# Splitting the raw weight blocks earlier and starting the block sums behind them, in a transformer kernel on one core

## What is computed

```python
def _moe_ref(x, w_in, w_out):          # w_in 512x2048, w_out 2048x512
    h = x @ w_in
    g = h - np.tanh(h)
    return g @ w_out

def _moe2_ref(x, w_in, w_out, g_ln):   # w_in 512x1024, w_out 1024x512
    h = x @ w_in
    e = np.exp(h - np.max(h, axis=-1, keepdims=True))
    solu = h * (e / (np.sum(e, axis=-1, keepdims=True) + 1e-09))
    mu, var = mean(solu), var(solu)    # over a row
    ln = (solu - mu) / np.sqrt(var + 1e-06) * g_ln
    return ln @ w_out
```

## Time and profile before

| | |
|---|---|
| median of 3 runs | 832.08 us (832.0 to 832.1) |
| the profiled execution | 825.32 us, its span 823.5 us |
| busy share of the span | PE 97%, PEld 84%, DVE 58%, ACT 48%, POOL 34% |
| granted TensorE clock, mean | 0.998 of full speed |

### The profile page before, as it was taken

One profiled execution on the slowest core, in us unless ns is written; L12 is line 12 of the kernel. 1 busy time (PEld: TensorE's weight loads), 2 busy tenths in 40 slices (PEclk: granted clock), 3 DMA queues, 4 the chain that ended last, 5 costly groups with the idle time before them and its releaser, 6 DMA issues. The chain is left out here.

```text
span 823.5 us, 14650 instructions
## 1 busy us (share of the span) xinstructions
PE 800.8 (97%) x4498; PEld 694.6 (84%) x4498; DVE 475.8 (58%) x1101; ACT 394.7 (48%) x935; POOL 280.3 (34%) x322
## 2 busy tenths in 40 slices
PE   6999999998999999999999999998999899999998
PEld 5888888887888888888888888897888788888886
DVE  5889888888854332233223322338678666666662
ACT  5999899888544332222222222325444443433433
POOL 3687787778100000000000000008274744444400
PEclk9999999999999999999999999999999999999999
DMA  7665555545433100000000000000200000000001
GB/s 184 149 154 159 143 137 154 144 114 145 138 113 110 65 1 0 1 1 0 0 0 0 0 0 0 0 1 1 102 1 1 27 25 27 14 25 25 13 25 51
DMA packets 77719, 46.34 MB, mean 56 GB/s; under 512 B 59824, under 2 KB 68144, under 8 KB 77680
## 3 DMA queue, kind: packets, MB, share of 16 engines
q1 hardware_dynamic: 75232, 45.19, 19.3%
q10 hardware_dynamic: 2448, 0.66, 0.4%
HBM read 40.97 MB, written 4.87 MB: 56 GB/s over the span
## 5 line engine op out<-in xcount | busy, mean ns | idle before, releaser
L1450 PE MATMUL psum<-x_hi,w1i 128*128 128x464 f32 (+1 forms) x640 | 185.7, 371 | 0.5 <-DVE w1i L1103 0.5
L1463 PE MATMUL psum<-gate_hi,w1o 128*128 128x464 f32 (+1 forms) x640 | 146.8, 371 | 3.3 <-DVE gate_lo L1146 3.3
L1463 PEld LDWEIGHTS psum<-gate_hi,w1o 128*128 128x128 f32 x640 | 119.9, 188 | 18.0 <-DVE gate_lo L1146 4.4
L1450 PEld LDWEIGHTS psum<-x_hi,w1i 128*128 128x128 f32 x640 | 119.7, 188 | 15.0 <-DVE w1i L1103 0.9
L1146 DVE TENSOR_TENSOR gate_lo<-gate,gate_hi 128x464 fp32r<-128x464 f32 (+1 forms) x80 | 56.4, 705 | 129.7 <-ACT gate_hi L853 129.7
L853 ACT ACTIVATE gate_hi<-gate 128x464 fp32r<-128x464 f32 (+1 forms) x80 | 47.1, 589 | 154.5 <-PE psum L1463 133.6
L706 POOL TENSOR_TENSOR w2t<-stage 128x512 f32<-128x512 f32 x2 | 4.8, 2442 | 338.0 <-PE psum L1463 338.0
L1450 PE MATMUL psum<-x_lo,w1i 128*128 128x464 f32 (+1 forms) x320 | 118.7, 371 | 0.0
L1134 DVE TENSOR_TENSOR gate<-psum,gate 128x464 f32<-128x464 f32 (+1 forms) x80 | 50.8, 636 | 94.2 <-ACT gate L840 94.1
L840 ACT ACTIVATE gate<-psum 128x464 f32<-128x464 f32 (+1 forms) x80 | 44.1, 551 | 101.7 <-PE psum L1450 97.2
L878 ACT ACTIVATE probs<-probs,neg_max 128x128 f32<-128x128 f32 (+2 forms) x144 | 83.7, 587 | 10.3 <-DVE neg_max L1179 10.0
(11 more groups left out here) (154 smaller groups left out, 1421.1 us busy)
## 6 DMA issues: line engine op xcount, KB each, us to landing
cum_bc<-cum_dram SPq DMA_DIRECT2D x16, 576.0 KB, 4.7
rden_T<-rden_dram SPq DMA_DIRECT2D x32, 144.0 KB, 3.0
out_x<-out_sb SPq DMA_DIRECT2D x18, 256.0 KB, 2.0
stage<-in_q SPq DMA_DIRECT2D x32, 128.0 KB, 2.4
v_raw<-in_v SPq DMA_DIRECT2D x32, 128.0 KB, 3.6
stage<-in_moe_w_in SPq DMA_DIRECT2D x16, 256.0 KB, 3.0
stage<-in_moe_w_out SPq DMA_DIRECT2D x16, 256.0 KB, 3.4
stage<-in_k SPq DMA_DIRECT2D x28, 128.0 KB, 2.3
```

Source lines behind the costliest of these rows:

```text
L1450: mm = pe.matmul(h_ps[j % 4][:, 0:wide(c)], wp[j][:, kt, :], xp[:, kt, 0:wide(c)], start=(n == 0), stop=(n == 3 * KT - 1))
L1463: mm = pe.matmul(y_ps[m][:, 0:wide(c)], wp[j][:, m * P:(m + 1) * P], gp[j % 2][:, 0:wide(c)], start=(j == 0 and wp is w1o_hi and gp is gat ...
```

## The change

The three raw blocks are split at steps 2, 3 and 5 of the last chunk, not 5, 6 and 7, and B11, B21 and T4 change slots so that each block's space is free by its step. POOL's sums get one more wait: until DVE has made the low parts of all three raw blocks. In the first rows of the second MLP, ACT does `exp2(1, 1)` ahead of `ln_hi(0, 1)`, and DVE does `solu(1, 0)` ahead of `ln_lo(0, 1)`.

```diff
-    W2_AT = {"B11": 0, "B21": 2, "T2": 4, "T1": 6, "T3": 8, "B22": 12, "T4": 14}
+    W2_AT = {"B21": 0, "T4": 2, "T2": 4, "T1": 6, "T3": 8, "B22": 12, "B11": 14}
-    W2_STEP = {"B22": 5, "B11": 6, "B21": 7, "T4": 9, "T2": 10, "T1": 11, "T3": 13}
+    W2_STEP = {"B22": 2, "B11": 3, "B21": 5, "T4": 9, "T2": 10, "T1": 11, "T3": 13}
...
             pool.wait_ge(down_done, FT * (NCH - 1) + 4)
+            pool.wait_ge(w2i_lo_done, 3)
             for kt in range(HK):
                 pool.tensor_tensor(sum_to("T1", kt), raw_half(kt, 1), raw_half(kt, 0), ALU.subtract).then_inc(w2_summed, 1)
...
             exp2(1, 0, 1)
+            exp2(1, 1, 1)
             ln_hi(0, 1)
-            exp2(1, 1, 1)
             normalise(1, 0)
...
             row_max(1, 1)
+            solu(1, 0, 1)
             ln_lo(0, 1)
-            solu(1, 0, 1)
             moments(1, 0)
```

## The result

| | before | the change |
|---|---|---|
| median | 828.19 us (17 runs, 825.24 to 834.31) | 824.69 us (17 runs, 821.42 to 826.46) |
| ratio, 95% interval | 1 | 0.9948 (0.9928 to 0.9969) |
| profiled execution, its span | 825.32 us, 823.5 us | 824.69 us, 822.9 us |
| mean granted clock of that execution | 0.998 | 0.994 |

The change is faster, by 0.5% (0.3% to 0.7%). The base moved too: the three runs of before at 832.0 to 832.1, on which the forecast was built, are not what before takes over 17 runs.

A forecast was written before the change was run, and what follows sets the result against it. PE, busy 97% of the span, was taken as the bound, so only its waits count: -3.34 us of stalls and +0.3 for the first rows make -3.0, from 832.08 to 829.0 us, range 828.2 to 830.6.

The forecast's parts named there:

- the base of the sum: The whole kernel: the predicted difference of -3.0 us was put on a median of 832.08 us, giving 829.0 us.
- -3.34 us for the stalls: Last chunk, down(5) to down(7): PE's waits for gate_lo, 0.66, 1.72 and 0.96 us, all go.
- three restarted groups: Groups of down behind the stalls: 1.87 against 1.81 us, worth 0.2 us, counted only in the forecast's low end.
- the tail, +0.3: First rows of the second MLP: the new order delays turn_ln(1, 0) by 0.3 us, range 0 to +1.9.
- balance of +0.36: Chain before turn_ln(1, 0): +0.4 for exp2(1, 1)'s start, +1.42 for its two halves, -1.46 for solu(1, 0).
- the splits: Raw splits at steps 2, 3 and 5: no work added, gate_lo done in time, all three stalls go, -3.34 us.
- rival 1: Last chunk: raw low parts are slow by themselves, 5.4 us a pair; 0.8 us come back, 829.8 us; chance 0.07.
- the slack: Steps 2, 3 and 5: gate_lo done 5.3 us after tanh, wanted by PE at 9.69, so 4.4 us spare.
- POOL's wait is free: Last chunk: POOL's first sum starts 2.1 us later, at 560.7, the eighth ends by 578.8; cost nothing.
- Rival 3: Step 9: the sums arrive late and ACT stands at T4, making the kernel slower, 833.8 us; chance 0.03.
- bound of 582.3: Step 9: PE begins to stall at down(9) only when POOL's sixth sum ends after 582.3 us.
- the second wait: First rows of the second MLP: PE waits 2.7 us on turn_ln(1, 0); expected to read 2.7 to 3.3 after.

The follow-up runs named there:

- experiment 2: The kernel before with only the new order of the first rows: 826.91 us, ratio 0.9998 to the kernel before.
- experiment 5: The changed kernel without POOL's added wait and with the first rows in the order of before: 822.85 us, ratio 0.9951 to the kernel before.
- experiment 4: The kernel before with POOL's added wait alone, raw splits still at steps 5, 6, 7: 827.09 us, ratio 0.9999 to the kernel before.
- experiment 6: The changed kernel with DVE's moments(1, 0) ahead of ln_lo(0, 1), ACT's order of before, POOL's rstd(1, 0) inside split_y(2, 0): 819.24 us, ratio 0.9905 to before.
- experiment 9: The kernel of experiment 6 with a small DMA holding up all of down(1), a 2.02 us pause: 822.55 us, ratio 0.9952 to the kernel before.
- experiment 1: The changed kernel with the first rows back in the order of before: 823.30 us, ratio 0.9953 to the kernel before.
- experiment 3: The kernel before once more, with no edit: 827.35 us, ratio 1.0004.
- experiment 8: The changed kernel once more, with no edit: 824.67 us, ratio 0.9965 to the kernel before.
- experiment 10: The kernel of experiment 6 with down(1) held behind its first four matmuls, a 1.12 us pause: 820.96 us, ratio 0.9929 to the kernel before.
- experiment 7: The kernel of experiment 6 with POOL's rstd(1, 0) left behind all of split_y(2, 0): 820.05 us, ratio 0.9916 to the kernel before.

## Why the prediction was wrong, and where it was right

**Wrong: the base of the sum.** The step was "on the median of the runs, 832.08 us, the same difference gives 829.0". Before takes 828.19 us over 17 runs, and 826.97, 826.21 and 826.89 in the later sets of 26, 29 and 11. The same difference of -3.0 on 828.19 gives 825.2, half a us from the result; that it comes so near is partly luck, since the next two errors go opposite ways. The profile held the hint: its own execution took 825.32 us at a clock of 0.998, and its distance of 6.76 us to the three runs was known, but the prediction carried the larger number on. How often the clock falls differs from run to run, so three runs that agree within 0.1 us do not make a base. Where those three lost their time stays open: their clock was not recorded, and no profile caught an execution of that length.

**Wrong in size: -3.34 us for the stalls.** The mechanism was right, and measured start to start the term is -4.1 (down(4) to down(8), 23.56 to 19.45 us). Summing the idle times left out 0.2 to 0.26 us at each of the stalls and 0.09 at down(8). The prediction saw part of this, "three restarted groups", and put 0.2 us for all three into the low end of its range only.

**Wrong in size: the tail, +0.3.** It measured +0.25 alone (experiment 2) and +0.66 in the change, inside the 0 to 1.9 that was given. Its balance of +0.36 is 0.44 by the rows. What the prediction named as a risk came on top: a small moments instruction of 0.57 us in the change, where it took 0.35 before and 0.15 in experiment 2. So the +0.25 that looks like the +0.3 is luck: nothing of the 0.44 overlapped, and the small instruction happened to come between two of POOL's. Together the measured terms make -4.1 + 0.66 = -3.4. The runs agree where the clock is equal: at a mean of 0.998, 23 runs of before have the median 825.40 and five of the change 821.79, a difference of 3.6.

**Right: the splits.** At 1.13 us a raw low part is 0.17 dearer than the 0.96 worked out from the turns, so rival 1 had a little of the truth; a pair of 2.27 still leaves the slack nearly whole, and its 5.4 us were due to the sums (experiment 5, 5.52). gate_lo(6), with both inputs in SBUF, takes 1.95 us beside a sum and nobody waits. The gate instruction (L1135), one of whose inputs is in PSUM, takes 0.62 us beside the same sums, as with POOL idle. So the sums go on blocking DVE instructions with two SBUF inputs and not all of DVE's, as the Trainium skill has it (SBUF — State Buffer, section Who interferes with whom).

**Right: POOL's wait is free, but only here.** tanh(5) comes 1.15 us later than in the profile of before; less that, the first sum starts at 561.3 us (predicted 560.7), the eighth ends at 577.1 (predicted: before 579), and w_out is loaded from 577.1 on. Rival 3 did not come in the change. Experiment 4 shows that it was near: 0.03 was fair for the change, but its bound of 582.3 counted instructions at their undisturbed lengths in the one place where the sums still run.

**Not foreseen: the price of the second wait.** The prediction took the 2.7 us on `turn_ln(1, 0)` as 2.7 us and asked only what the change adds. By experiment 6 it is more: from pair 1 to `turn_ln(1, 0)` that kernel takes 20.45 us, 2.8 less than before and 3.4 less than the change, and where the clock falls behind the wait, the 1.5 us of that go too.

## What to carry to other kernels

Price a stall of PE from the start of one group to the start of the next, against a pair of groups that did not stall; the idle time in the row was a lower bound here, and by the granted clock of the rows behind it one sees whether the clock fell as well. Before a sum is put on a base, ask whether that base and the profiled execution are the same kind of run: their distance, and the mean clock of each run, are worth more than three runs that agree. And where two engines take turns, a bound must use the lengths that instructions have beside each other.

## What the runs showed of the hardware

- **A pause of PE can cost its clock.** Behind the pauses of 2.02 (experiment 9) and 2.84 us (the change) PE ran for some us at a mean of 0.57 to 0.72 of full speed and lost about 1.6 us more. The wait on `turn_ln(1, 0)`, 2.5 to 2.9 us in experiments 1 to 5 and 8, cost 1.4 to 1.6 us more in the same way, and the clock fell behind the 2.33 us of experiment 4 too. Behind pauses of 0.66 to 1.72 (before), 1.12 (10) and 0.68 us (7) it did not fall. But the length of one pause does not settle it. Behind the same wait, 2.70 us in the first profile of before, the clock was full, and in experiment 3, the same kernel, it was not. And near 203 us it fell in three of the 13 profiles (the change, experiments 5 and 10) behind two waits of 0.5 and 1.3 us with 0.5 us of work between them; in the other ten, with the same two waits, it did not. What decides between them stays open.
- **Reading with a step seems dearer on DVE.** One raw low part of 512 elements, read with a step of eight words and with POOL idle, takes 1.13 us; gate_lo, 448 contiguous elements, takes 0.62, and the low part of a sum, 1024 contiguous ones, 1.23. That the step is the reason is argued from this, not tried.
- **DVE and POOL take turns by whole instructions.** gate_lo takes 0.62 us with POOL idle and up to 2.40 beside a sum (experiment 4), where it ends with the sum or behind it; the gate instruction, which reads PSUM and one SBUF tile, takes 0.62 in both.
